# Open-expert weight loads, small choice steps, weight splits and the scatter end moved to other places in a fused attention, MoE and FFN kernel

## The reference

```python
keep = is_sink | in_window
scores = np.where(keep, scale * q @ k.T, -1e9)
a = softmax(scores)
x = (a @ v)                                   # as [3072 tokens, 512]
logits = x @ w_gate + modality_bias[modality_id]
e_idx = argmax(logits)                        # top-1 of 8 experts
out[mask] = gate_w * (relu(x[mask] @ w1[e]) @ w2[e])   # 512 -> 1024 -> 512
h = out @ w_in                                # 512 -> 2048
return (h * sigmoid(1.702 * h)) @ w_out
```

## Time and profile before

| | us |
|---|---|
| median of 3 runs | 1119.61 |
| lowest, highest | 1116.31, 1120.78 |
| the profiled execution | 1116.31 |
| its span in the trace | 1114.5 |
| TensorE busy in it | 1095.8 (98%) |
| GpSimd, VectorE, ScalarE busy | 353.7, 429.1, 385.9 |
| mean granted clock of TensorE | 0.994 |

### The profile page before, as it was taken

One profiled execution on the slowest core, in us unless ns is written; L12 is line 12 of the kernel. 1 busy time (PEld: TensorE's weight loads), 2 busy tenths in 40 slices (PEclk: granted clock), 3 DMA queues, 4 the chain that ended last, 5 costly groups with the idle time before them and its releaser, 6 DMA issues.

```text
span 1114.5 us, 18600 instructions
## 1 busy us (share of the span) xinstructions
PE 1095.8 (98%) x5883; PEld 936.9 (84%) x5884; DVE 429.1 (38%) x1109; ACT 385.9 (35%) x798; POOL 353.7 (32%) x492
## 2 busy tenths in 40 slices
PE   9999999989899999999999999999999999999998
PEld 8999999978688888888888888888888888888887
DVE  5666666657322233121265223222322222222222
ACT  3666666744221233122253222222222222222222
POOL 8899999972446413121120001001001001000100
PEclk9999999989999999999999999999999999999999
DMA  9998899315821123121133101000100000000101
GB/s 225 231 244 212 227 229 247 108 46 182 288 89 38 47 88 147 47 76 46 38 113 115 29 1 47 19 9 38 28 9 38 19 19 32 6 0 0 39 1 39
DMA packets 59700, 96.27 MB, mean 86 GB/s; under 512 B 8192, under 2 KB 33024, under 8 KB 59648
## 3 DMA queue, kind: packets, MB, share of 16 engines
q1 hardware_dynamic: 53888, 76.75, 25.1%
q0 software_dynamic: 5760, 18.89, 4.9%
HBM read 76.21 MB, written 19.41 MB: 86 GB/s over the span
## 4 chain that ended last, share of the span: by engine, by line
PE 88%; POOL 5%; DVE 2%; issue 2%; ACT 1%; DMA 1%; POOLq 0%; DVEq 0%; ACTq 0%
PE psum L1264 8%; PE psum L1265 8%; PE psum L1266 8%; PE psum L1257 8%; PE psum L1256 8%; PE psum L1255 8%; PE psum L970 4%; PE psum L1195 4%; PE psum L1198 4%; PE psum L1201 4%; PE psum L1164 4%; PE psum L1168 4%; PE psum L1172 4%; PE psum L945 2%; PE psum L1183 2%
## 5 line engine op out<-in xcount | busy, mean ns | idle before, releaser
L2041 DVE TENSOR_TENSOR g<-psum,g 128x512 f32<-128x512 f32 x96 | 66.3, 691 | 291.9 <-ACT g L1485 291.9
L1485 ACT ACTIVATE g<-psum 128x512 f32<-128x512 f32 x96 | 57.3, 598 | 305.4 <-PE psum L1257 304.6
L1264 PE MATMUL psum<-w_hi,gT_hi 128*128 128x512 f32 x384 | 151.4, 394 | 0.0
L902 POOL DMA_INDIRECT out<-o_out,out_rows x20 | 19.3, 964 | 411.9 <-ACT o_out L1505 407.3
L1265 PE MATMUL psum<-w_lo,gT_hi 128*128 128x512 f32 x384 | 149.7, 390 | 0.0
L1266 PE MATMUL psum<-w_hi,gT_lo 128*128 128x512 f32 x384 | 149.7, 390 | 0.0
L1255 PE MATMUL psum<-x2T,win_hi 128*128 (+1 forms) x384 | 149.6, 390 | 0.0
L1257 PE MATMUL psum<-x2T,win_lo 128*128 (+1 forms) x384 | 149.6, 389 | 0.0
L1256 PE MATMUL psum<-x2T,win_hi 128*128 (+1 forms) x384 | 149.4, 389 | 0.0
L970 PE MATMUL psum<-v_sb,pT 128*128 128x73 f32 x704 | 107.9, 273 | 4.3 <-DVE v_sb L1813 2.3
L970 PEld LDWEIGHTS psum<-v_sb,pT 128*128 128x128 f32 x704 | 95.3, 194 | 11.2 <-DVE pT L1777 6.2
(11 more groups left out here) (312 smaller groups left out, 1894.6 us busy)
## 6 DMA issues: line engine op xcount, KB each, us to landing
qk_raw<-qkT SPq DMA_DIRECT2D x64, 384.0 KB, 7.5
stage<-w SPq DMA_DIRECT2D x12, 1024.0 KB, 8.3
x<-y_rows SPq DMA_DIRECT2D x24, 256.5 KB, 2.6
vT_sb<-vT SPq DMA_DIRECT2D x16, 384.0 KB, 5.0
v_sb<-vP SPq DMA_DIRECT2D x16, 384.0 KB
x_rows<-x_sb SPq DMA_DIRECT2D x16, 384.0 KB, 3.7
win_raw<-w SPq DMA_DIRECT2D x16, 256.0 KB, 4.2
win_raw<-w_in SPq DMA_DIRECT2D x16, 256.0 KB, 6.6
```

The source lines that it names most:

```text
L1264: pe.matmul(psum[:, OB[t], :], gh, hi, start=(f == 0), stop=False)
L2041: dve.tensor_tensor(g32[:, f % 2, :], psum[:, FB[f % 2], :], g32[:, f % 2, :], ALU.mult)\
```

## The change

Places are moved; no arithmetic changes.

- SyncE starts with the loads of the open expert's weights in pair 7 instead of 6, so every pair of parts is loaded one pair of heads later.
- ScalarE casts part j at step 104 + 6 j for all 16 parts; before, parts 10 to 15 came at steps 161, 164, 170, 173, 182 and 185.
- In batch 1, VectorE's steps n = 12, 18, 22, 23, 24 of the open choice become 9, 16, 18, 19, 20, and ScalarE's `o_exps` goes from n = 20 to 14. GpSimd's `open_choice` goes from behind head 16 to behind head 17.
- In batch 3, VectorE's routing steps 35, 38, 44, 45, 46 become 36, 39, 45, 46, 47; ScalarE's gate exponentials go from 41 to 42 and TensorE's `rank_early` from 43 to 44.
- On GpSimd, of the three `split_open` ahead of `below` one stays there; the other two and the two ahead of the marks go behind the marks. The wait for scores in `gather_open` names an earlier step.
- On GpSimd, the wait for the end of an open scatter stands right behind its issue (so for tile 0 ahead of `gather(1)`), and `finish_scatter` goes ahead of `gather(2)`.

```diff
--- before.py
+++ after.py
@@ -57,7 +57,7 @@
     TURN_LAG, PV_LAG = 3, 4
     TAIL = PV_LAG + 1
     VW_AT, VW_MOVE = 1, 3
-    EXP_AT, RANK_AT_STEP = 41, 43
+    EXP_AT, RANK_AT_STEP = 42, 44
     WARM_UP = 7
     OPEN_RANK_STEP, OPEN_INV_STEP = 29, 16
     CH = DM // P
@@ -66,7 +66,7 @@
     GT = BANK // P
     GROUPS = NTILE // GT
     LEAD = 4
-    OPEN, OPEN_LOAD = 2, 6
+    OPEN, OPEN_LOAD, OPEN_HEAD = 2, 7, 17
     OPEN_PARTS, OPEN_BACK, WIN_AT = 16, 21, 2
     OPEN_RANK, OPEN_INV, OWN_INV = 448, 504, 384
     YW = DM + 1
@@ -413,8 +413,6 @@
 
         TURN_AFTER = {5 + 2 * t: t for t in range(GT)}
 
-        cast_at = {n: j for j, n in enumerate([104 + 6 * j for j in range(10)] + [161, 164, 170, 173, 182, 185])}
-
         def open_part(j):
 
             q, c = divmod(j, 4)
@@ -745,7 +743,7 @@
 
             def gather_open():
 
-                pool.wait_ge(scores_ready, (B - 1) * HT + 6 * QT)
+                pool.wait_ge(scores_ready, (B - 1) * HT + 2 * QT)
                 for c in range(PAIRS):
                     pool.wait_ge(x_stored[c], DMA * 2)
                 for t in range(OPEN):
@@ -754,7 +752,7 @@
                                             bass.IndirectOffsetOnAxis(open_gather[:, t:t + 1], 0))\
                         .then_inc(open_gathered[t], 16)
 
-            between = {9: make_biases, 11: open_logits, 12: open_ties, 13: open_chain, 16: open_choice,
+            between = {9: make_biases, 11: open_logits, 12: open_ties, 13: open_chain, 17: open_choice,
                        18: open_marks, 25: open_rows}
             for h in range(1, B * H):
                 split_qk(*divmod(h, SLOT))
@@ -766,8 +764,7 @@
             pool.wait_ge(logits_added, B - 1)
             pool.tensor_tensor(lg[:, 0:PRE, :], lg[:, 0:PRE, :], bias_of[:, 0:PRE, :], ALU.add).then_inc(pre_biased, 1)
 
-            for j in range(B * H - OPEN_BACK, OPEN_PARTS - 2):
-                split_open(j)
+            split_open(B * H - OPEN_BACK)
             pool.wait_ge(best_found, 1)
             pool.tensor_tensor(below[:, 0:PRE, :], lg[:, 0:PRE, :], col(best[:, 0:PRE], some), ALU.subtract)\
                 .then_inc(shifted, 1)
@@ -799,13 +796,14 @@
             then(pool.tensor_copy(seen[:, PRE, :], batch_sum[:, B - 2, :]))
             pool.sem_inc(tiles_seen, 1)
 
-            for j in range(OPEN_PARTS - 2, OPEN_PARTS):
-                split_open(j)
             pool.wait_ge(rows_known, 1)
             pool.wait_ge(scores_ready, (B - 1) * HT + 42)
             for t in range(PRE):
                 pool.tensor_scalar(oh_slot[:, t, :], iota_row[:], rank_p[:, t:t + 1], None, ALU.is_equal)\
                     .then_inc(rows_marked, 1)
+            for j in range(B * H - OPEN_BACK + 1, OPEN_PARTS):
+                split_open(j)
+
             def finish_scatter():
 
                 t0, t1, t2, t3 = (tokens[:, k, :] for k in range(4))
@@ -861,19 +859,15 @@
                 pool.wait_ge(y_moved, t + 1 + PRIMED)
                 pool.indirect_dma_start(y_dram, bass.IndirectOffsetOnAxis(open_scatter[:, t:t + 1], 0),
                                         open_ys[:], None).then_inc(scattered, 16)
-
-            def end_open(t):
                 pool.wait_ge(scattered, t * 16 + 16)
                 pool.sem_inc(rows_written, 1)
 
             gather(0)
             scatter_open(0)
             gather(1)
-            end_open(0)
+            finish_scatter()
             gather(2)
-            finish_scatter()
             scatter_open(1)
-            end_open(1)
             pool.wait_ge(runs_ready, 1)
             total = pool.value_load(table[0:1, TOTAL:TOTAL + 1], min_val=NTILE - 4 - OPEN, max_val=SLOTS - 4) + 4
             for t in range(WIN_AT + QUARTERS):
@@ -1369,11 +1363,14 @@
                     pack_sinks(b, n // QT - 1)
                 if n < HT and n % (2 * QT) == VW_AT:
                     spread_sinks(b, n // (2 * QT))
-                if b == 1 and n == 3 * QT + 2:
+                if b == 1 and n == 2 * QT + 2:
                     act.wait_ge(open_shifted, 1)
                     act.activation(o_exps[:], o_below[:], ACT.Exp).then_inc(open_exped, 1)
-                if n < HT and b * HT + n in cast_at:
-                    round_open(cast_at[b * HT + n])
+                j = (b * HT + n - 2) // QT - OPEN_HEAD
+                if n % QT == 2 and 0 <= j < OPEN_PARTS and (n < HT or b == B - 1):
+                    if j * BANK >= HALVES - QT * P - BANK:
+                        act.wait_ge(open_inverted, 1)
+                    round_open(j)
                 if b == B - 1 and n == EXP_AT:
                     gate_exps(slice(0, PRE), 1)
                 if b == B - 1 and n == HT + 2:
@@ -1382,8 +1379,6 @@
             def round_open(j):
 
                 q, cols = open_part(j)
-                if (j + 1) * BANK > HALVES - QT * P:
-                    act.wait_ge(open_inverted, 1)
                 act.wait_ge(open_loaded[j // 2], 32)
                 act.copy(win_hi[:, q, cols], win_raw[:, q, cols]).then_inc(open_high, 1)
 
@@ -1677,18 +1672,18 @@
 
                 ranks = psum[:, VW_ps, OPEN_RANK:OPEN_RANK + QT * E].rearrange("p (t e) -> p t e", e=E)
                 counts = psum[:, VW_ps, OPEN_RANK + QT * E:OPEN_RANK + (QT + 1) * E]
-                if n == 12:
+                if n == 9:
                     dve.wait_ge(open_biased, 1)
                     dve.tensor_reduce(o_best[:], o_lg[:], AX.X, ALU.max).then_inc(open_best, 1)
-                if n == 18:
+                if n == 16:
                     dve.wait_ge(open_tied, 1)
                     dve.tensor_reduce(o_lead[:], o_tied[:], AX.X, ALU.max).then_inc(open_lead, 1)
-                if n == 22:
+                if n == 18:
                     dve.wait_ge(open_exped, 1)
                     then(dve.tensor_reduce(o_gate[:], o_exps[:], AX.X, ALU.add))
-                if n == 23:
+                if n == 19:
                     then(dve.tensor_scalar(o_gate[:], o_gate[:], 1e-9, None, ALU.add))
-                if n == 24:
+                if n == 20:
                     dve.reciprocal(o_gate[:], o_gate[:]).then_inc(open_gated, 1)
                 if n == OPEN_RANK_STEP + 2:
                     dve.wait_ge(open_ranked, 1)
@@ -1732,19 +1727,19 @@
                 if n == 30:
                     dve.tensor_scalar(seen[:, QT:PRE:QT, :], row(from_end[:], [P, B - 2, E]), 0.0, None, ALU.mult)\
                        .then_inc(seen_cleared, 1)
-                if n == 35:
+                if n == 36:
                     dve.wait_ge(pre_biased, 1)
                     dve.tensor_reduce(best[:, pre], lg[:, pre, :], AX.X, ALU.max).then_inc(best_found, 1)
-                if n == 38:
+                if n == 39:
                     dve.wait_ge(ties_marked, 1)
                     dve.tensor_reduce(lead[:, pre], tied[:, pre, :], AX.X, ALU.max).then_inc(lead_found, 1)
                 if n == 37:
                     then(dve.tensor_tensor(lower[:], e_col, e_row, ALU.is_gt))
-                if n == 44:
+                if n == 45:
                     make_gates(pre, 1)
-                if n == 45:
+                if n == 46:
                     take_ranks(pre, psum[:, VW_ps, 0:PRE * E].rearrange("p (t e) -> p t e", e=E), 1)
-                if n == 46:
+                if n == 47:
                     whole_tiles(pre)
                     rows_in_tile(pre).then_inc(rows_known, 1)
                 if n == HT:
```

## The result

The changed kernel takes 1167.42 us (median of 4 runs, 1163.16 to 1172.04), the kernel before 1118.39 beside it. The ratio is 1.0438, 95% interval 1.0391 to 1.0487: 49 us slower. The prediction said slower, and 1134. The profiled execution took 1160.31 us with a span of 1158.5, 44.0 more than before.

The account below looks back on a forecast made before the run. The prediction took TensorE, busy for 98% of the span, to set the pace: 1116.3 + 15.7 + 2.0 + 2.5 + 0.5 - 9.1 - 2.4 + 5 = 1130.5, with 3.3 of the median 1134 us; range 1125 to 1146.

Parts of the forecast that it names:

- What bounds the kernel, and the sign: Whole kernel: TensorE is busy 98%, so only its standstill or lower clock counts; the change makes it slower.
- Part 1: Attention: late weight loads make ScalarE's cast wait and stop TensorE, 15.7 us in six pairs plus 2.0 in two.
- rival A: Late weight loads land in 2.6 us, stop TensorE 1.2 each, 9.6 in eight pairs; about 1121; chance 0.15.
- rival C: Late weight loads land early enough to cover ScalarE's wait; only Part 3 and Part 4 stay; about 1111; chance 0.05.
- The Trainium skill's 3.2 us: Open expert's weight loads: both parts land 3.2 us behind first issue, TensorE stops 1.1 us per pair, sum 9 us lower.
- The lower clock: Attention: three of six gaps of about 2.6 us followed by a low stretch, 1.6 us each: +5 (0 to 24).
- Rival B: In attention, clock falls after every gap: 24 us instead of 5, some 1153; sign granted clock under 0.9; chance 0.12.
- Part 2: Open choice's moved steps: VectorE waits for GpSimd's open_choice, 2.5 us lost, plus 0.5 for the o_best read and o_exps.
- Part 3: End of attention: GpSimd's splits behind the marks and later routing steps win back all 9.1 us (0 to -9.1).
- Part 4: First expert tiles: finish_scatter ahead of gather 2, new gap of 2.4 us there, less at gather 3; -2.4 (-6.4 to +2).
- The sum: Whole kernel: all terms added to the profiled 1116.3 give 1130.5, with the 3.3 of the median 1134.

Follow-up runs that it names:

- Experiments 3 and 4: Changed kernel with 20 (3) or nine (4) further identity matmuls on TensorE in each of the eight places where it stands still: 1156.17 and 1147.06 us.
- undo_choice: Changed kernel with the steps of the open choice (VectorE, ScalarE, GpSimd) back as before: 1163.40 us, ratio 1.0413.
- one_late: Kernel before with one of the eight pairs of weight loads a pair of heads later: 1120.72 us, ratio 1.0014.
- experiments 5 to 7: 5: changed, ScalarE's casts two steps later, 1141.32 us; 6: before, one load pair late, 1120.72 us; 7: before, three load pairs late, 1132.90 us.
- experiment 12: Kernel before with five splits ahead of the marks, last batch's routing one step later, scatter_open(1) ahead of finish_scatter: 1111.58 us, ratio 0.9931.

## Why the prediction was right and wrong, by its steps

- **What bounds the kernel, and the sign: right.** Time was lost where TensorE stood still or ran low: 37.5 us by the end of attention and 6.5 in the first expert tiles.
- **Part 1, the late loads: the mechanism right, the gaps well sized.** 17.7 us of gaps were forecast, 15.4 came. ScalarE's mean wait was 3.4 us (27.5 over 8) against 3.9 for six pairs and 2.3 for two. Landings had a median of 4.1 us, as before, so rival A and rival C fell. The Trainium skill's 3.2 us for both parts fell too; its section, Anatomy of one DMA, gives that fit for transfers that GpSimd issues, and these are SyncE's.
- **The lower clock: the step that failed.** The forecast put +5 us here: three of six gaps followed by a stretch of 3.4 us at 1.6 each. Five of seven were followed by one, 3.4 to 13.7 us long, 51.2 us in all, 24.5 us lost. The mistake was to take the shorter of the two stretches that the trace before showed, though its longer one, 10.4 us, followed a gap of 2.3 us in attention's last two heads, and to give it to half of the gaps alone. Rival B, with a chance of 0.12, used the longer one: 24 us for this term, where 24.5 came. That its 1153 is still 14 us under the measured median is due to parts 3 and 4, 10.8 us short, and to the profiled run, which is faster than the others. The mean clock of 0.70 and 0.68 in the windows above is the sign that the prediction had named for B. Experiments 3 and 4 show the clock's part by filling the gaps with work.
- **Part 2, the open choice: nearly right.** 3.0 us were forecast. VectorE waited 2.88 us at `o_row`, TensorE 2.88, and with the short low stretch behind it TensorE is 3.9 later from step 90 to 96. The other 0.9 of the 4.8 in the table were there at step 90, and they are not shown to be the change's: 0.3 stand at the first step of all, and `undo_choice` and `one_late`, which keep the old steps, are 0.5 later at step 90 as well. Undoing it gave 4.0, within the scatter.

```profile
119.77 0.20 DVE L1701 TENSOR_REDUCE o_row<-o_rank 128x6 f32<-128x48 f32 x1 [2.88 <-POOL o_rank L711]
...
121.95 0.67 PE L964 MATMUL psum<-v_sb,pT 128*128 128x73 f32 x4 [2.88 <-DVE pT L1772]
```

- **Part 3, GpSimd at the end of attention: right at first, wrong in what it covers.** Of 9.1 us, 7.2 came back in attention; 1.2 us of the wait before `rank_early` stayed. "The four moved splits fit between the marks and the first gather" looked at GpSimd's idle time alone and missed VectorE beside it: 4.4 us of its routing, 3.1 us of TensorE, and 3.4 us of low clock from 297 us on.
- **Part 4: the gain didn't come.** -2.4 was forecast for it; alone it measures +0.11%, from -0.01 to +0.23%. `finish_scatter` took 7.9 us (321.33 to 329.2) where 7.5 were forecast, but gather 2 landed 7.4 us after its issue, beyond the 6.1 that was the upper bound, and TensorE stood 5.8 us, with 6.8 us of low clock around it. In the chain of waits:

```profile
326.76 2.42 POOL scatter_i L820
329.25 0.57 issue
329.99 7.39 DMA xs<-x_rows,gather_i
337.43 1.11 PE psum L1049 x4
```

- **The sum.** Put together from what was measured, with the clock at 24.5 instead of 5, parts 3 and 4 at what they gave (-7.2 + 6.5 for all of the first expert tiles instead of -11.5), part 1 at 15.4 and part 2 at 4.8, the trace's 1116.3 becomes 1160.3. That is the profiled execution's own time, as it must be, since the terms are its lateness taken apart. The medians differ by 5 us more than the profiled executions; the changed kernel's runs scatter over 9 us, and the profiled one is faster than all of them.
- **Left open.** How long the clock stays low behind a gap. Stretches of 3.4 to 17 us followed gaps of like length, and experiments 5 to 7 didn't find what decides. It could not be said beforehand from one trace to better than the two ends, 1.6 and 4 or more us a gap.

## What to carry to other kernels

Where a matrix engine is full, price a repeated gap at its length plus the lower clock behind it, and take the longest low stretch that the trace shows after a like gap, not the shortest; here the second part was 1.6 times the first. A load that is issued by an event of the same stage a few steps ahead of its use has to be early by its landing time, and the one constant that moves it cost 46.5 us here, where all fine placement of experiment 12 won 7.6. Before work is moved into an engine's idle time, look at which engine it would hold up then.

## What the hardware showed that I had not expected

- Gaps of TensorE from 2.1 to 3.3 us in the same stage were followed by 0, 3.4, 10.2 or 13.7 us at 1.2 GHz, and once a gap of 1.47 us by 10.2 us. Nine matmuls of the identity per gap (2.2 us) left one low stretch, of 10.2 us, where the changed kernel had five behind such gaps.
- A 0.18 us VectorE `tensor_tensor` on 128 x 24 elements, and in another run a 0.36 us one on 128 x 192, took 4.58 and 5.27 us beside four back-to-back GpSimd `tensor_tensor`s of 1.24 us each; beside GpSimd's 18 `tensor_scalar`s of 0.6 us, just before, the one on 128 x 192 took 0.36 us in the kernel before and 0.42 in the changed one.
- The other way round, two GpSimd operations of `finish_scatter` on 128 x 32 elements took 2.4 us each instead of 0.4, each beside one of VectorE's `w_lo` of 2.29 us.
